# Fourth x casts moved to the middle of a unit, shares moved a unit later, row-sum epsilon moved to ScalarE: an attention + expert + SoLU kernel

## The chip, the cores and the metric

The kernel runs on one core of a Trainium2 chip. The metric is the device time of one execution in microseconds (us), lower is better. TensorE does the matrix products, VectorE and ScalarE read its results from PSUM, GpSimd works on SBUF alone, and SyncE issues all of the transfers.

## The reference

Three stages, in fp32, one behind the other. Batch 4, 8 heads, 576 positions, head size 64; so 2304 tokens of width 512.

```python
# attention, block-causal with blocks of 64
scores = scale * q @ k.T ; scores = where(block_i >= block_j, scores, -1e9)
attn = exp(scores - max) ; attn = attn / (sum(attn) + 1e-9) ; x = attn @ v
# four experts, F = 1024, weighted by normalised shares
p = domain_probs / (domain_probs.sum(-1) + 1e-9)
for e in range(4): out += p[:, e:e+1] * (relu(x @ w1[e]) @ w2[e])
# SoLU layer
h = x @ w_in ; solu = h * softmax(h) ; ln = layernorm(solu) * g_ln ; out = ln @ w_out
```

## The kernel before

**Numbers in two parts.** Every operand of a matrix product is held as a high part (a cast, made by ScalarE in most places) and a low part (value less high part, made by GpSimd or VectorE). A product is then three matmuls: high x high, low x high, high x low.

**Attention.** 16 steps, one for each pair of heads. In step p TensorE turns (transposes) the exponentials of pair p, multiplies them by the values, and makes the scores of pair p + 1. VectorE takes the row maxima, the low parts of the turned tiles, and scales the outputs of pair p - 1 by the inverse row sums (`scale_right`, `scale_left`). ScalarE takes the exponentials (each of the nine row blocks leaves its row sums in one column of `sums`, read back by a small instruction of its own behind the exponential) and the high parts. The inverse sums go this way: `floor_sums` adds 1e-9 to `sums` (L1217), `invert_sums` takes the reciprocal into `rinv_wide` (L1221), TensorE turns `rinv_wide` behind the second turned tile (T8R, L1598), ScalarE copies it out (`copy_rt`, L915), SyncE stores it and loads it back spread over all partitions as `r_sb`, which the scaling waits for. On VectorE the order at the start of step p is `floor_sums(p)`, `scale_right(p - 1, .., 0)`, `invert_sums(p)`, then the maxima of block 8. On ScalarE a step ends with the exponentials of blocks 2, 3 and 0 and `late(p)`, which holds a cast of w1 or x in some steps; the next begins with the high part of the first turned tile (T8) and `copy_rt`.

**Experts.** 4 experts x 3 groups of 768 tokens (sg) x 4 quarters of F (u) = 48 units, m = 0 to 47. The up product of a unit is a Strassen-like scheme of seven products `m1, m6, m2, m7, m5, m4, m3` (6 matmuls each); each takes one sum of w1 and one sum of x (B21, B22, B11, T3, T1, T2, T4), and their results are combined by VectorE and ScalarE into c11, u2, u3, c22, c21, c12. In program order TensorE does m1, m6, m2 of unit m, the four down products of unit m - 1 (36 matmuls), then m7, m5, m4, m3 of unit m. `m6` of the next unit waits until c12 is combined, `m2` for ScalarE's copy of m1 (`m1_copied`; the tiles are `m_a` and `m_b`), `m4` until u3 is there. On VectorE c12 comes behind the low part of c22, and that behind ScalarE's high part of c22.

**The sums of x.** They are made once for each sg and both halves t, in four rounds r of one or two sums: (B21, B22), (B11, T3), (T1, T2), (T4). GpSimd joins x (`x_join`, L761) and adds (`x_add`, L773 to L781); ScalarE casts the high parts of a round (`x_cast`, L935, L948); GpSimd makes the low parts (`x_low_part`, L785). For sg = 0 they are written to `xr` at once. For sg = 1 and 2 they go to one of two buffers `x_tmp` (by r % 2), SyncE stashes them in HBM (`stash_round`, L552) and a cast into a buffer waits until the stash before it has landed (`tmp_stored`). At the start of each sg, SyncE loads the seven sums back into `xr` (`load_operands`, L559), one by one, in the order of the products, each when its stash has landed and the product of the unit before has read the old one. SyncE works through one list in order: (1,0) rounds 0 and 1, w2 loads, the stashes of sg 0's own sums (`stash_first`, seven of 768 KB, in two lots), (1,0) rounds 2 and 3, the rows of x for (2,0), (1,1) rounds 0 to 3, the loads for unit 4, the rows for (2,1), the eight stashes of sg 2, the loads for unit 8.

**Where the casts stand before.** In ScalarE's program for a unit, e = 0, sg < 2: u = 1 behind the copy of c11: (sg+1, 0) rounds 0 and 1. u = 2 behind the copy of m1: (sg+1, 0) rounds 2 and 3; u = 2 at the end: (sg+1, 1) rounds 0 and 1. u = 3 behind the copy of m1: (sg+1, 1) rounds 2 and 3. `after_c11` (L1064) makes the w2 casts of the unit first.

**The shares.** `normalise_probs` (L1353): seven small VectorE operations on 128x18 to 128x72 values, each waiting for the one before, in unit 1 between the w2 low parts and u3. `accumulate` reads the shares from unit 4 on.

Of the kernel before, what the change touches and what calls it, by code (L numbers as in the profile page):

```python
# [16 lines left out]
def build_program(nc, q, k, v, domain_probs, w1, w2, w_in, w_out, g_ln, out):  # L17
# [3 lines left out]
    ALU = mybir.AluOpType  # L21
    ACT = mybir.ActivationFunctionType
# [23 lines left out]
    EPS = 1e-9  # L46
    LN_EPS = 1e-6
    SCALE = 1.0 / DH ** 0.5
    BLOCKS = SEQ // BLOCK
# [92 lines left out]
    with ctx:  # L142
# [78 lines left out]
        sums = put("sums", [P, BLOCKS])  # L221
        sums_e = put("sums_e", [P, BLOCKS])
# [101 lines left out]
        exped = sem("exped")  # L324
# [3 lines left out]
        sums_ready = sem("sums_ready")  # L328
        rinv_made = sem("rinv_made")
# [566 lines left out]
        def _(act):  # L896
            def exp_scores(b, n):
                act.wait_ge(maxed, BLOCKS * n + through_group(group_no(b)))
                if not (isinstance(n, int) and n == 0):
                    act.wait_ge(turned, NT * (n - 1) + last_turn(b) + 1)  # L900
                    if b == 8:
                        act.wait_ge(sums_ready, n)
                target = pr[b][:, 0:keys(b)]
                if b == 8:
                    target = target.rearrange("p (b x) -> p b x", b=2)
                act.activation(target, score_view(b), ACT.Exp, bias=neg_max[:, score_no(b):score_no(b) + 1],  # L906
                               accum_out=sums[:, b:b + 1]).then_inc(exped, 1)

            def high(i, p, par):
                act.wait_ge(turned, NT * p + i + 1)  # L910
                act.activation(turn_target(i, 0), turn_source(i, par), ACT.Copy).then_inc(high_done, 1)
# [65 lines left out]
            def late(p):  # L977
                if p in (0, 2, 4, 6):
                    w1_cast_plain(0, p // 2, 1)
                if p == 11:  # L980
                    x_cast(0, 0, 3)
                if p in (13, 14):
                    x_cast(0, 1, 3 * (p - 13))

            def step(p, par, ahead=True):
                n = p + 1
                high(T8, p, par)
                copy_rt(p, par)
                high(T8R, p, par)
                exp_scores(8, n)  # L990
                high(T67, p, par)
                middle(p)
                high(T67B, p, par)
                exp_scores(7, n)
                high(T45, p, par)
                exp_scores(6, n)
                high(T452, p, par)
                nearly_late(p)
                exp_scores(5, n)
                if ahead:  # L1000
                    key_high(p + 2, par)
                exp_scores(1, n)
                exp_scores(4, n)
                high(T0123, p, par)
                exp_scores(2, n)
                exp_scores(3, n)
                exp_scores(0, n)
                late(p)

            def last_step(p, par):  # L1010
# [27 lines left out]
            key_high(1, 1)  # L1038
            for b in SCORE_ORDER:
                exp_scores(b, 0)  # L1040
            for p in range(PAIRS - 1):
                step(p, p % 2, ahead=p < PAIRS - 2)
            last_step(PAIRS - 1, 1)
# [20 lines left out]
            def after_c11(e, sg, u):  # L1064
                nx = next_w2(e, sg, u)
                if nx:
                    split2(nx[0], 2 * nx[1], gained=nx[0] == EXPERTS)
                    split2(nx[0], 2 * nx[1] + 1, gained=nx[0] == EXPERTS)
                if e == 0 and sg < 2 and u == 1:
                    x_cast(sg + 1, 0, 0)  # L1070
                    x_cast(sg + 1, 0, 1)
                nx = next_w1(e, sg, u)
                if nx:
                    w1_cast_sums(*nx)

            def unit(e, sg, u):
                m = HALF_F * (SUPERS * e + sg) + u
                if m >= 1:
                    copy_m1(m)
                    after_m1(e, sg, u)  # L1080
                hid_c11(m)
                if m >= 1:
                    after_c11(e, sg, u)
                hid_rest(m, "c22", 2, u3[:, :])
                hid_rest(m, "c21", 1, m1(m))
                hid_rest(m, "c12", 3, u2[:, :])
                if e == 0 and sg < 2 and u == 2:
                    x_cast(sg + 1, 1, 0)
                    x_cast(sg + 1, 1, 1)

            for e in range(EXPERTS):
                for sg in range(SUPERS):
# [105 lines left out]
        def _(dve):  # L1198
# [15 lines left out]
                                         in1=k_h[slot][:, :].bitcast(f32), op0=ALU.mult, op1=ALU.subtract  # L1214
                                         ).then_inc(k_split, 1)

            def floor_sums(p):  # L1217
                dve.wait_ge(exped, BLOCKS * (p + 1))
                dve.tensor_scalar(sums_e[:, :], sums[:, :], EPS, None, ALU.add).then_inc(sums_ready, 1)

            def invert_sums(p):  # L1221
                dve.wait_ge(sums_ready, p + 1)
                dve.reciprocal(rinv_wide[:, 0:BLOCKS], sums_e[:, :]).then_inc(rinv_made, 1)  # L1223
# [16 lines left out]

            def step(p, par, first=False, ahead=True):
                n = p + 1
                floor_sums(p)
                if not first:
                    scale_right(p - 1, 1 - par, 0)
                invert_sums(p)
                max_scores(8, n)
                low(T8, p, par)
                if not first:
                    scale_right(p - 1, 1 - par, 1)  # L1250
                low(T8R, p, par)
                max_scores(7, n)
                if not first:
                    scale_left(p - 1, 1 - par)
                low(T67, p, par)
                max_scores(6, n)
                low(T67B, p, par)
                max_scores(5, n)
                low(T45, p, par)
                max_scores(1, n)  # L1260
                max_scores(4, n)
                low(T452, p, par)
                max_scores(2, n)
                max_scores(3, n)
                if ahead:
                    key_low(p + 2, par)
                max_scores(0, n)
                low(T0123, p, par)
# [53 lines left out]
                dve.tensor_tensor(u3[:, :], bank_y(m), m1(m), ALU.add).then_inc(comb_done, 1)  # L1322

            def last_step(p, par):
                floor_sums(p)
                scale_right(p - 1, 1 - par, 0)
                invert_sums(p)
                low(T8, p, par)
                scale_right(p - 1, 1 - par, 1)
                low(T8R, p, par)  # L1330
                scale_left(p - 1, 1 - par)
                low(T67, p, par)
                low(T67B, p, par)
                low(T45, p, par)
                make_u2(0)
                low(T452, p, par)
                low(T0123, p, par)
                scale_right(p, par, 0)
                scale_right(p, par, 1)
                split2(0, 0)  # L1340
                split2(0, 1)
# [40 lines left out]
            def unit(e, sg, u):  # L1382
                n = SUPERS * e + sg
                m = HALF_F * n + u
                if m >= 1:
                    make_u2(m)
                if n >= 1 and u == 1:
                    accumulate(n - 1, 1, downs(m - 2, 4))
                hid_low(m, "c11", 0, bank_x(m))
                nx = next_w2(e, sg, u)  # L1390
                if nx and m >= 1:
                    split2(nx[0], 2 * nx[1], gained=nx[0] == EXPERTS)
                    split2(nx[0], 2 * nx[1] + 1, gained=nx[0] == EXPERTS)
                if n >= 1 and u == 0:
                    if n == 1:
                        for i in range(2):
                            dve.wait_ge(x_stored[i], 16 * PAIRS)
                    if n == 2:
                        dve.wait_ge(x_low, NR * 2 * SUPERS)
                        for s in range(2):  # L1400
                            dve.wait_ge(tmp_stored[s], 16 * 4 * (SUPERS - 1))
                    accumulate(n - 1, 0, downs(m - 1, 2))
                if m == 1:
                    normalise_probs()
                make_u3(m)
                if m == 0:
                    scale_left(PAIRS - 1, 1)
                dve.wait_ge(prod_done, made(m, "m5"))
                dve.wait_ge(comb_done, combined(m, "u3"))
                dve.tensor_tensor(u3[:, :], bank_x(m), u3[:, :], ALU.add).then_inc(comb_done, 1)  # L1410
                dve.wait_ge(prod_done, made(m, "m4"))
                dve.tensor_tensor(m1(m), bank_y(m), m1(m), ALU.add).then_inc(comb_done, 1)
                hid_low(m, "c22", 2, u3[:, :])
                dve.wait_ge(prod_done, made(m, "m3"))
                dve.tensor_tensor(u2[:, :], bank_x(m), u2[:, :], ALU.add).then_inc(comb_done, 1)
                hid_low(m, "c21", 1, m1(m))
                hid_low(m, "c12", 3, u2[:, :])
# [535 lines left out]
```

## Time and profile before

| | us |
|---|---|
| median of 3 runs | 1171.48 (1171.28 to 1173.45) |
| profiled execution, its own time | 1173.69 |
| its span | 1171.9 |
| TensorE busy | 1143.4 (98%) |
| VectorE busy | 645.2 (55%) |
| ScalarE busy | 425.4 (36%) |
| GpSimd busy | 414.7 (35%) |
| granted clock, mean | 0.997 |

Busy time is an average over stages: in the attention stage (up to about 190 us) all four engines are busy most of the time, behind it TensorE alone is. In the rows, PE is TensorE, PEld its weight loads, DVE VectorE, ACT ScalarE, POOL GpSimd, SP SyncE with its DMA queue. Times are us from the start of the span.

### The profile page before, as it was taken

To read this page: it belongs to the slowest core of one execution; us is meant where nothing else is said; L and a number is where in the kernel's file an instruction comes from. 1 tells how busy PE (TensorE), PEld (TensorE's weight loads), DVE (VectorE), ACT (ScalarE), POOL (GpSimd) and SP (SyncE) were. 2 spreads that over 40 slices of the span, in tenths; PEclk is the share of its full clock that TensorE was granted. 3 is DMA by queue.
4 is the path that set the end of the run, shared out by engine and by line. 5 is a ranking of instruction groups with operands and counts; after the bars stand their busy time and mean duration, and the time that the engine had idled before them with its cause. 6 is when DMAs were issued, how large, how long until landed. Compare 5 with 4: busy or idle time off the path is not lost.

```text
span 1171.9 us, 16745 instructions
## 1 busy us (share of the span) xinstructions
PE 1143.4 (98%) x6131; PEld 1021.0 (87%) x6131; DVE 645.2 (55%) x1155; ACT 425.4 (36%) x927; POOL 414.7 (35%) x403
## 2 busy tenths in 40 slices
PE   8999998989989999999999999999999999999998
PEld 7999888879879999999999999999999987888887
DVE  8999997634234533334443434343434368766775
ACT  7888885222213211113321112321112344434432
POOL 7998896652424300004400003410002454442330
PEclk9999999999999999999999999999999999999999
DMA  4766666983472304071504043422225100000000
GB/s 140 218 206 198 211 228 199 368 309 143 143 270 101 142 17 172 1 260 55 207 1 188 1 160 119 151 92 81 109 81 198 37 18 10 28 19 27 19 27 36
DMA packets 68341, 146.28 MB, mean 125 GB/s; under 512 B 6064, under 2 KB 34736, under 8 KB 68272
## 3 DMA queue, kind: packets, MB, share of 16 engines
q1 hardware_dynamic: 68272, 145.36, 35.7%
q8 instruction: 43, 0.70, 0.3%
q14 instruction: 26, 0.21, 0.1%
HBM read 114.60 MB, written 30.74 MB: 124 GB/s over the span
## 4 chain that ended last, share of the span: by engine, by line
PE 75%; DVE 1%; POOL 1%; DMA 1%; issue 0%; ACT 0%; ACTq 0%; POOLq 0%
PE s L1724 34%; PE outp L1585 19%; PE s L1585 10%; PE ring L1585 10%; PE ring L1855 1%; PE s L1798 1%; DMA xr<-x_stash 1%; POOL x_late L761 0%; DMA x_stash<-x_tmp 0%; POOL yop_l L863 0%; DVE yop_l L1433 0%; ACT y_t L1103 0%; DVE acc L1379 0%; POOL x_tmp L785 0%; DVE ex L1505 0%
## 5 line engine op out<-in xcount | busy, mean ns | idle before, releaser
L1724 PE MATMUL s<-xr,w1s 128*128 128x384 f32 x2016 | 363.4, 338 | 11.2 <-issue 6.3
L1724 PEld LDWEIGHTS s<-xr,w1s 128*128 128x128 f32 x2016 | 352.8, 189 | 17.8 <-issue 7.9
L1053 ACT ACTIVATE hid_h<-u 128x384 fp32r<-128x384 f32 x96 | 50.5, 526 | 375.6 <-DVE u L1410 350.6
L720 POOL TENSOR_TENSOR work<-work 128x256 f32<-128x256 f32 x20 | 15.9, 796 | 395.2 <-DMA work<-in_moe_w 269.3
L1365 DVE SCALAR_TENSOR_TENSOR hid_l<-s,hid_h 128x384 fp32r<-128x384 f32 x48 | 26.8, 557 | 134.4 <-ACT hid_h L1049 134.4
L1724 PE MATMUL s<-w1s,yop_h 128*128 128x512 f32 x252 | 85.7, 399 | 1.8 <-POOL yop_l L863 0.7
L1049 ACT ACTIVATE hid_h<-s 128x384 fp32r<-128x384 f32 x48 | 23.5, 490 | 154.9 <-PE s L1585 154.9
L1585 PE MATMUL s<-k_h,qb 128*128 128x288 f32 (+8 forms) x320 | 75.8, 324 | 3.9 <-ACT pr L906 1.9
L1322 DVE TENSOR_TENSOR u<-s,m_b 128x384 f32<-128x384 f32 x24 | 13.4, 558 | 118.7 <-PE s L1724 118.7
L906 ACT ACTIVATE pr<-s,neg_max 128x576 f32<-128x576 f32 (+2 forms) x144 | 75.5, 534 | 4.6 <-DVE neg_max L1201 4.4
L1585 PE MATMUL outp<-w_h,hid_h 128*128 128x512 f32 x192 | 75.4, 393 | 0.0
L1585 PE MATMUL s<-w_h,hid_h 128*128 128x512 f32 x192 | 75.2, 392 | 0.0
L1585 PE MATMUL s<-w_l,hid_h 128*128 128x512 f32 x192 | 75.0, 391 | 0.0
L1585 PE MATMUL outp<-w_l,hid_h 128*128 128x512 f32 x192 | 74.9, 390 | 0.0
L1585 PE MATMUL s<-w_h,hid_l 128*128 128x512 f32 x192 | 74.7, 389 | 0.0
L1585 PE MATMUL ring<-w_h,hid_h 128*128 128x512 f32 x192 | 74.7, 389 | 0.0
L1585 PE MATMUL ring<-w_h,hid_l 128*128 128x512 f32 x192 | 74.7, 389 | 0.0
L1585 PE MATMUL ring<-w_l,hid_h 128*128 128x512 f32 x192 | 74.7, 389 | 0.0
L1585 PE MATMUL outp<-w_h,hid_l 128*128 128x512 f32 x192 | 74.6, 389 | 0.0
L1596 PE MATMUL ring<-ident,pr 128*128 128x128 f32 x400 | 64.9, 280 | 5.8 <-DVE rinv_wide L1223 4.8
L1322 DVE TENSOR_TENSOR u<-s,m_a 128x384 f32<-128x384 f32 x24 | 13.4, 558 | 97.1 <-PE s L1724 97.1
L1201 DVE TENSOR_REDUCE neg_max<-s 128x1 f32<-128x576 f32 (+2 forms) x144 | 65.3, 473 | 0.9 <-PE s L1585 0.8
(172 smaller groups left out, 2455.8 us busy)
## 6 DMA issues: line engine op xcount, KB each, us to landing
xr<-x_stash SPq DMA_DIRECT2D x77, 768.0 KB, 6.3
r_sb<-r_scratch SPq DMA_DIRECT2D x16, 576.0 KB, 4.2
x_rows<-x_n SPq DMA_DIRECT2D x32, 288.0 KB, 4.6
work<-x_rows SPq DMA_DIRECT2D x24, 384.0 KB, 6.6
x_stash<-x_tmp SPq DMA_DIRECT2D x12, 768.0 KB, 3.9
work<-in_moe_w SPq DMA_DIRECT2D x32, 256.0 KB, 4.2
stage<-in_moe_w SPq DMA_DIRECT2D x32, 256.0 KB, 5.0
x_stash<-xr SPq DMA_DIRECT2D x7, 768.0 KB, 9.6
```

The source lines that it names most:

```text
L720: pool.tensor_tensor(s1, a21, a22, ALU.add).then_inc(w1_sums, 1)
L906: act.activation(target, score_view(b), ACT.Exp, bias=neg_max[:, score_no(b):score_no(b) + 1], accum_out=sums[:, b:b + 1]).then_inc(exped, 1)
L1049: act.activation(hid[0][0][:, :], bank_x(m), ACT.Relu).then_inc(hid_high, 1)
L1053: act.activation(hid[slot][0][:, :], source, ACT.Relu).then_inc(hid_high, 1)
L1201: dve.tensor_reduce(neg_max[:, score_no(b):score_no(b) + 1], score_view(b), AX.XY if b == 8 else AX.X, ALU.max, negate=True).then_inc(maxe ...
L1322: dve.tensor_tensor(u3[:, :], bank_y(m), m1(m), ALU.add).then_inc(comb_done, 1)
L1365: dve.scalar_tensor_tensor(out=hid[slot][1][:, :], in0=source, scalar=0.0, in1=hid[slot][0][:, :].bitcast(f32), op0=ALU.max, op1=ALU.subtr ...
L1585: last = pe.matmul(target, x, y, start=start and i == 0, stop=stop and i == 2)
L1596: last = pe.transpose(slot[:, at * P:(at + 1) * P], pr[b][:, j * P:(j + 1) * P], ident[:, :])
L1724: last = pe.matmul(target, x, y, start=start and i == 0, stop=stop and i == 2, skip_group_check=True)
L1798: last = pe.transpose(s01[:, 512 * i + d * P:512 * i + (d + 1) * P], acc[:, t * D + d * P:t * D + (d + 1) * P], ident[:, :])
L1855: last = pe.transpose(ring[:, f * P:(f + 1) * P], ex[i % 2][:, f * P:(f + 1) * P], ident[:, :])
```

## The change

Three moves; every operation is still done as often as before.

```diff
@@ ScalarE, attention
+            def floor_sums(p):
+                act.wait_ge(exped, BLOCKS * (p + 1))
+                if not (isinstance(p, int) and p == 0):
+                    act.wait_ge(rinv_made, p)
+                act.activation(sums_e[:, :], sums[:, :], ACT.Copy, bias=EPS).then_inc(sums_ready, 1)
@@ def step: behind exp_scores(0, n), ahead of late(p); and once behind the first pair's exponentials
+                floor_sums(n)
@@ ScalarE, after_c11
-                if e == 0 and sg < 2 and u == 1:
-                    x_cast(sg + 1, 0, 0)
-                    x_cast(sg + 1, 0, 1)
+                if e == 0 and sg < 2 and u in (1, 2):
+                    x_cast(sg + 1, u - 1, 0)
+                    x_cast(sg + 1, u - 1, 1)
@@ ScalarE, end of unit
-                if e == 0 and sg < 2 and u == 2:
-                    x_cast(sg + 1, 1, 0)
-                    x_cast(sg + 1, 1, 1)
@@ VectorE, attention
-            def floor_sums(p):
-                dve.wait_ge(exped, BLOCKS * (p + 1))
-                dve.tensor_scalar(sums_e[:, :], sums[:, :], EPS, None, ALU.add).then_inc(sums_ready, 1)
@@ VectorE, first line of step and of last_step
-                floor_sums(p)
@@ VectorE, unit
-                if m == 1:
+                if m == 2:
                     normalise_probs()
```

## Rows read from the trace of the kernel before

**Rows 1.** Stretches: each engine's busy us (instructions), granted clock, DMA share, GB/s.
```profile
326.00:328.00 2.00, 2.00 (x7) 1.63 (x7) 0.00 (x0) 0.49 (x1) 0.00 (x0) 0.50 1.03 430
420.00:1105.00 685.00, 682.56 (x3410) 605.51 (x3409) 323.83 (x559) 186.07 (x327) 150.05 (x155) 1.00 0.24 87
```
**Rows 2.** Who waited for whom, whole span: us in total, times, longest.
```profile
PE s L1724 <- issue: 6.3, 2, 3.7
PE ring L1596 <- DVE rinv_wide L1223: 4.8, 8, 1.1
PE s L1724 <- ACT m_b L1027: 1.9, 2, 1.0
```
**Rows 3.** Chain that ended last, 195 to 420 us: start, us, what.
```profile
242.45 3.78 POOL x_late L761 x3
...
251.65 6.15 DMA xr<-x_stash
...
269.71 7.28 PE s L1724 x42
...
321.55 3.74 issue
325.29 5.05 PE s L1724 x18
...
369.50 7.28 PE s L1724 x42
...
384.98 7.30 PE s L1724 x42
```
**Rows 4.** Timeline, units 2 to 4: start, us, engine, line, what [idle before, releaser].
```profile
232.41 6.40 PE L1724 MATMUL s<-xr,w1s 128*128 128x384 f32 x36
...
235.28 0.53 ACT L1053 ACTIVATE hid_h<-u 128x384 fp32r<-128x384 f32 x1 [7.20 <-DVE u L1410]
...
237.79 1.56 ACT L948 ACTIVATE x_tmp<-x_late 128x768 fp32r<-128x768 f32 x2
...
238.70 3.62 POOL L785 TENSOR_TENSOR x_tmp<-x_late,x_tmp 128x768 fp32r<-128x768 f32 x2 [7.04 <-ACT x_tmp L948]
...
239.78 1.31 PE L1724 MATMUL s<-xr,w1s 128*128 128x384 f32 x6 [0.97 <-ACT m_b L1027]
...
257.85 3.69 PE L1724 MATMUL s<-xr,w1s 128*128 128x384 f32 x12 [0.55 <-DMA xr<-x_stash]
```
**Rows 5.** Timeline of ScalarE, unit 6.
```profile
303.38 0.53 ACT L1053 ACTIVATE hid_h<-u 128x384 fp32r<-128x384 f32 x1 [8.24 <-DVE u L1410]
...
305.89 1.56 ACT L948 ACTIVATE x_tmp<-x_late 128x768 fp32r<-128x768 f32 x2
```
**Rows 6.** The two stashes (1, 0) of rounds 2 and 3, by tile.
```profile
L555 SPq DMA_DIRECT2D x_stash<-x_tmp x2: 370/566/761, 225.6 to 226.6; - x2
...
DMA to landing us min/median/max: 11.1/11.1/11.1
```
**Rows 7.** Timeline, unit 1: the shares and what follows.
```profile
214.12 4.12 DVE L1360 TENSOR_TENSOR probs_n<-probs_raw,probs_sum 128x18 f32<-128x18 f32 x4
...
218.89 5.48 PE L1724 MATMUL s<-xr,w1s 128*128 128x384 f32 x30 [1.21 <-DVE u L1322]
```
**Rows 8.** Timeline of the attention stage, at the epsilon and the inverses.
```profile
26.15 0.27 ACT L915 ACTIVATE rt_sb<-ring 9x128 f32<-9x128 f32 x1 [0.53 <-PE ring L1598]
...
128.54 0.49 DVE L1238 TENSOR_TENSOR x_n<-outp,r_sb 128x320 f32<-128x320 f32 x1 [0.54 <-DMA r_sb<-r_scratch]
...
173.87 1.85 POOL L785 TENSOR_TENSOR xr<-t_first,xr 128x768 fp32r<-128x768 f32 x1
...
173.93 1.82 DVE L1219 TENSOR_SCALAR sums_e<-sums 128x9 f32<-128x9 f32 x1 [0.46 <-ACT pr L906]
...
176.41 0.30 PE L1596 MATMUL ring<-ident,pr 128*128 128x128 f32 x1 [0.79 <-DVE rinv_wide L1223]
...
189.77 1.29 PE L1724 MATMUL s<-xr,w1s 128*128 128x384 f32 x6 [0.91 <-POOL xr L785]
```

More of the change, by code:

```diff
@@ L1040, in _ @@
                 exp_scores(b, 0)
+            floor_sums(0)
             for p in range(PAIRS - 1):
@@ L1324, in last_step @@
             def last_step(p, par):
-                floor_sums(p)
                 scale_right(p - 1, 1 - par, 0)
```

## The prediction, made before the changed kernel was seen

> **What bounds the kernel now.** I read the stretches first. From 420 to 1105 us TensorE is busy 682.56 of 685 us at the full clock [rows 1]: nothing that this change touches can shorten the work there, and one unit of the expert stage is 15.48 us (384.98 less 369.50) [rows 3]. So the change can only win or lose where TensorE waits. The list of TensorE's waits gives those places [rows 2]: 6.3 us in two idle times with no visible releaser, 4.8 us for the inverted sums (`rinv_wide`) in the attention stage, 1.9 us in two waits for a ScalarE copy `m_b`. The chain of waits places the first: the operand loads at the starts of units 4 and 8, each of which hangs on a line cast of x -> GpSimd's low parts -> stash -> reload [rows 3]. The granted clock is the last view: at 326 to 328 us it is 0.50, the 1.2 GHz level [rows 1], after an idle time of 3.74 us.
>
> What the two restarts cost, before: at unit 4, 0.97 us for `m_b` [rows 4], 0.55 us before the second product, 2.57 us before the first (6.3 less 3.74 [rows 2, 3]; unit 3 had ended at 253.45), and 12 matmuls in 3.69 us. At the full clock 12 take 2.08; the lower clock costs 1.6. At unit 8: the other 0.9 of the `m_b` waits [rows 2], 3.74 idle, and 18 matmuls in 5.05 where 3.12 is due: 1.9. That is 5.7 and 6.6 us [rows 2 to 4]. (A stretch of the chain with 42 matmuls is 7.28 us, so one is 0.173.)
>
> **The change part by part.**
>
> (a) *The fourth pair of x casts (sg+1, t=1, rounds 0 and 1) goes from the end of unit 2 to its middle*, behind the two w2 casts and ahead of the three hidden copies. Work is the same: two casts in 1.56 us [rows 4]. What matters is when its semaphores come, and what is queued behind it on ScalarE, which works in order.
>
> At the second restart (unit 6, making x for unit 8) the middle is free: ScalarE waits 8.24 us for the hidden copy at 303.38, and the casts come at 305.89 [rows 5]. The cast needs the stashes of rounds 2 and 3 landed; these are issued near 293.5 and 294.6 and a stash takes 3.6 to 5.6 us there, so about 297 to 300. The casts are then done by 299 to 301, before ScalarE is wanted. GpSimd's 3.6 us of low parts, the stashes, the round-2 cast in unit 7 (which waited for a stash until 314.3) and the loads all move up by some 6 us; the first operand is in by about 317 and the second by 319 to 321, where TensorE comes for them at 320.3 and 321.3. I take all three items as gone: -6.6. The bounds are -6.9 (with the slow restart after each idle time) and -4 (the second operand about a microsecond late, and the clock falls anyway).
>
> At the first restart (unit 2, making x for unit 4) the middle is not free. The cast of round 0 needs the stash of (1, 0, 2) and that of round 1 the stash of (1, 0, 3). They are issued at 225.6 and 226.6 and land 11.1 us later each, at 236.7 and 237.7 [rows 6], as they stand behind seven 768 KB stashes. Before, the casts started at 237.79, past both; now ScalarE stops at the first of them from about 227 on. The copy of c22, which it made at 235.28 [rows 4], is behind it in the queue. With the 1.2 us of (b) TensorE is earlier: unit 3 starts at 232.41 + 24 x 0.173 = 236.57 before, 235.3 now, and its first product ends at 236.4. Its second (`m6`) needs c12, which VectorE adds only after c22's low part. The chain: cast 236.7 to 237.5, cast 237.7 to 238.5, copy of c22 to 239.05, low part to 239.6, c12 to 240.1 (each of the three some 0.55 us). So TensorE, which lost 0.97 us here, now idles about 3.7 us. That is as long as the 3.74 us that pulled the clock to 0.50 [rows 1, 3], so I count a fall here: +1.9. Unit 3's remaining work, from 241.0 to 253.45 before (12.4 us), starts at 242.2: it ends at 254.6, or 256.5 with the lower clock.
>
> And the loads? GpSimd gets the round-0 cast at 237.6 instead of 238.70 [rows 4], 1.1 us earlier; the chain from there (join of x at 242.45, last load 251.65 to 257.80 [rows 3]) moves by as much, the second operand lands at 256.7. TensorE, held up, arrives at 256.5, wants it at 257.6 and does not wait; no fall of the clock there. Unit 5 starts at 256.5 + 15.48 = 272.0, before it was 269.71 + 4.16 = 273.87 [rows 3]: -1.9 with (b) in it. If the clock does not fall in unit 3, the landing at 256.7 decides: 256.7 + 14.4 = 271.1, -2.8. If it falls twice: 0.
>
> (b) *The shares (`normalise_probs`) go from unit 1 to unit 2.* In unit 1 four of its seven small operations take 4.12 us and TensorE waits 1.21 us for the u3 behind them [rows 7]. In unit 2 VectorE starts them near 228.5; GpSimd's 1 us sums of x end at 231.7 and then GpSimd has nothing until the casts. I expect the shares done near 232.5, u3 started as its product comes, no wait. Gain in unit 1: 1.2, already spent in (a), where what comes next is late; bounds 0 and 1.3 for that term.
>
> (c) *The epsilon of the row sums goes from VectorE to ScalarE*, 16 times. Before: the last exponential's sum is read, VectorE adds (0.17 us where nothing is beside it, up to 1.82), scales (0.48), inverts (0.20), and TensorE waits 0.79 us at 176.41 [rows 8]. Now VectorE scales before the sums are there; ScalarE adds in some 0.3 us: the nearest row is its copy of 9x128, 0.27 us [rows 8], plus its wait for its own last write. The inversion comes 0.25 to 1.9 us earlier. Of TensorE's eight waits [rows 2] (0.40, 0.49, 0.47, 1.09, 0.34, 0.33, 0.79, 0.91 in order; one stands in [rows 8]), those at 129.3 and 164.3 stay, since the scaling, at 128.54, waited for the loaded inverses (`r_sb`) [rows 8]. The last two (0.79, 0.91) give nothing: from 166 us on GpSimd works without a pause to the last low part of x, for which the first expert product waits at 189.77 [rows 8]; TensorE would only wait longer there. That leaves 0.40 + 0.49 + 0.47 + 0.34 = 1.7: -1.7. On ScalarE the add costs about 0.3 us and the sum's read-back; behind it are the late cast and the copy of the first turned tile, and then ScalarE idles anyway for the inverses' transpose, 0.53 us at the least [rows 8]. Bounds: -4.8 (all of [rows 2]'s item) and +4.8 (16 x 0.3, if nothing covers it). I take -1.7, near the rows that say who waits.
>
> The 1.82 us add at 173.93 ran while GpSimd had a 1.85 us operation from 173.87, and ended just behind it [rows 8]. The Trainium skill (SBUF — State Buffer, section SBUF: two separate sides) says that VectorE in a two-port mode and GpSimd lock one pair of ports for whole instructions, while ScalarE never waits for anyone. By that rule the add's long forms vanish on ScalarE and don't pass on to the inversion; my sum has it so, and without it the inversion would inherit some of the delay, about -1. Against the move, the Trainium skill (ScalarE: Activation LUTs, Rules for kernel authors) says to put `add` on VectorE, not ScalarE; what that would do is rival D.
>
> **Sum**, against the profiled execution (span 1171.9, its own time 1173.7): -6.6 - 1.9 - 1.7 = -10.2: span 1161.7, time 1163.5. The median of the runs, 1171.48, is 2.2 below that execution; the same difference from it gives **1161.3 us**.
>
> **Rivals.**
>
> A. *The block in unit 2 is mild, or the attention stage gains all.* No fall of the clock there (-0.9) and up to -3 more from (c): 1157.5 to 1160.4. For: the first fall came behind two idle times with one product between; attention's slow steps are slow on VectorE too. Against: 3.7 us is as long as the idle time before the second fall.
>
> B. *The block costs more than it gives*: a second fall at unit 4, or landings a microsecond later: the first restart gives 0 or loses 1, with the rest as forecast: 1163.2 to 1164.3. For: the DMA engines are full there, the landing is fixed by them and not by ScalarE.
>
> C. *The second restart keeps half of its wait*: the second operand comes late and the clock falls: -4 in place of -6.6, or -2: 1163.9 to 1165.9. Against: nothing else is in the DMA queue there.
>
> D. *Slower: ScalarE becomes the attention stage's bound.* Place: between the last exponential and the copy of the turned inverses. Price: wait for its own sum (0.4, what VectorE waited for it), the add 0.27 and a lost overlap of 0.1, 0.75 us a step, in 15 steps 11.3 us; with -8.5 from the rest and nothing of the -1.7: 1174.3. It decides where ScalarE's idle time before the inverses is under 0.75 us; the smallest is 0.53 [rows 8], but most steps have over 1.
>
> E. *Nothing of (a) arrives*: if the operand loads' start is set by the order on SyncE's queue and not by the casts, only (c) stays: 1169.8. Against: the chain [rows 3] runs through the GpSimd join and the stash.
>
> **How the numbers follow.** Forecast 0.50, A 0.22, B 0.12, C 0.09, D 0.04, E 0.03. Range 1157 to 1165.5: it takes in A, B, and most of C. 0.2% is 2.3 us, about what a measurement of this kernel can tell: all but D, and a mix of E with losses (0.01), are faster. Faster 0.94, same 0.02, slower 0.04.
>
> **What would show it.** Right: no idle time of TensorE at units 7 and 8, no 0.50 clock there; the casts of unit 6 near 299 less the shift; in unit 2 ScalarE waiting for `x_stash<-x_tmp` to about 236 and TensorE idle 3 to 4 us before `m6` of unit 3, with a fall of the clock behind it; no wait for u3 in unit 1 or 2; TensorE's wait for `rinv_wide` at 2 to 3.5 us, and a longer one for x before the first expert product. Wrong: idle time on TensorE before the first product of unit 4 or 8 of over 1 us; ScalarE never idle before the inverses' transpose; steps of the attention stage longer than the 11.1 us of the quick ones now.

## The result, and the profile after

The changed kernel took 1159.86 us in the median of 4 runs (1159.10 to 1160.79), the kernel before 1172.30 us in 4 runs beside it (1171.28 to 1173.45): a ratio of 0.9894, 95% interval 0.9877 to 0.9911. A second set of 4 runs gave 0.9887 (0.9867 to 0.9908). The forecast was 1161.3 us, range 1157 to 1165.5.

The profiled execution took 1159.74 us, its span is 1157.9; TensorE is busy 1138.7 us, VectorE 633.4, ScalarE 428.5, GpSimd 415.7, mean granted clock 0.999. The span is 14.0 us shorter, the median 12.4: the execution that the prediction was made against was among the longer ones of its kernel.

The chain of waits from 195 us on (start, us, what), which answers to [rows 3]:

```profile
235.37 4.24 POOL x_late L761 x3
...
241.44 3.55 DMA x_stash<-x_tmp
...
245.44 7.41 DMA xr<-x_stash
...
262.41 7.28 PE s L1723 x42
277.89 7.28 PE s L1723 x42
...
308.85 7.30 PE s L1723 x42
324.34 7.28 PE s L1723 x42
```

One row of 42 matmuls stands for one unit. They now follow each other every 15.48 us right through units 7 and 8, where before 3.74 us of issue and a slow stretch lay between. Three marks divide the gain: A, the start of the first expert product (the last row of [rows 8], 189.77 before); R5, the first row of 42 matmuls in this chain (269.71 before; unit 5 starts 4.16 behind it); R9, the same one turn later (338.54 before, 324.34 now).

| | before | after | change | forecast |
|---|---|---|---|---|
| A (attention) | 189.77 | 185.31 | -4.46 | -1.7 |
| A to R5 (first restart, shares) | 79.94 | 77.10 | -2.84 | -1.9 |
| R5 to R9 (second restart) | 68.83 | 61.93 | -6.90 | -6.6 |
| sum | | | -14.20 | -10.2 |

The list of TensorE's waits, whole span (us in total, times, longest), answers to [rows 2]: the issue and `m_b` lines are gone, a new one leads.

```profile
PE s L1723 <- DVE u L1414: 2.5, 1, 2.5
PE ring L1595 <- DVE rinv_wide L1224: 1.7, 3, 0.9
...
PE ring L1595 <- DVE ptr_l L1213: 1.6, 2, 0.9
...
PE s L1723 <- POOL xr L785: 1.5, 1, 1.5
```

The timeline of units 2 to 4 (start, us, engine, line, what, idle before and releaser) shows where the new wait comes from; it answers to [rows 4, 7].

```profile
223.43 0.22 DVE L1355 TENSOR_REDUCE probs_sum<-probs_raw 128x18 f32<-128x72 f32 x1
...
224.75 1.41 DVE L1359 TENSOR_TENSOR probs_n<-probs_raw,probs_sum 128x18 f32<-128x18 f32 x4
...
226.19 5.37 PE L1723 MATMUL s<-xr,w1s 128*128 128x384 f32 x30
227.50 0.56 DVE L1322 TENSOR_TENSOR u<-s,m_a 128x384 f32<-128x384 f32 x1 [1.33 <-PE s L1723]
...
230.41 1.79 ACT L954 ACTIVATE x_tmp<-x_late 128x768 fp32r<-128x768 f32 x2 [8.55 <-DMA x_stash<-x_tmp]
...
232.10 0.51 ACT L1061 ACTIVATE hid_h<-u 128x384 fp32r<-128x384 f32 x1
...
232.64 0.92 DVE L1364 SCALAR_TENSOR_TENSOR hid_l<-u,hid_h 128x384 fp32r<-128x384 f32 x1 [2.58 <-ACT hid_h L1061]
233.48 0.55 DVE L1414 TENSOR_TENSOR u<-s,u 128x384 f32<-128x384 f32 x1
...
234.08 3.76 PE L1723 MATMUL s<-xr,w1s 128*128 128x384 f32 x12 [2.53 <-DVE u L1414]
```

The last four of the shares' seven operations take 1.41 us in place of 4.12, and no TensorE wait for u3 follows. ScalarE stands 8.55 us at the moved casts, with the copy of c22 (232.10) behind them; VectorE has to wait for that copy (2.58), c12 comes at 233.48, and TensorE idles 2.53 us before `m6`. That is the block forecast in step (a), and the clock falls behind it, as the stretches show (columns as in [rows 1]):

```profile
234.00:236.00 2.00, 1.92 (x6) 1.92 (x7) 2.00 (x3) 0.90 (x2) 1.87 (x2) 0.50 0.99 356
236.00:238.00 2.00, 2.00 (x10) 1.95 (x9) 1.76 (x2) 0.85 (x1) 2.00 (x2) 0.71 1.02 369
326.00:328.00 2.00, 2.00 (x14) 2.00 (x13) 1.06 (x3) 0.52 (x1) 0.00 (x0) 1.00 0.12 43
```

The attention stage, as the stretch 5 to 185 us (before, then after):

```profile
5.00:185.00 180.00, 170.84 (x1276) 159.41 (x1274) 168.82 (x340) 149.36 (x438) 154.73 (x141) 1.00 0.63 197
```

```profile
5.00:185.00 180.00, 171.76 (x1298) 162.72 (x1297) 162.65 (x332) 155.56 (x465) 159.73 (x144) 1.00 0.65 202
```

VectorE is busy 6.2 us less, ScalarE 6.2 more, and TensorE has issued 22 more matmuls by the same moment. The add by tile (ns min/median/max), before and after, with the inversion after:

```profile
L1219 DVE TENSOR_SCALAR sums_e<-sums x16: 174/608/1820, 13.4 to 186.4; 128x9 f32<-128x9 f32 x16
```

```profile
L913 ACT ACTIVATE sums_e<-sums x16: 211/212/213, 13.4 to 181.9; 128x9 f32<-128x9 f32 x16
L1224 DVE RECIPROCAL rinv_wide<-sums_e x16: 204/215/219, 13.6 to 182.2; 128x9 f32<-128x9 f32 x16
```

On VectorE the add took anything from 0.17 to 1.82 us; on ScalarE it takes 0.21 each time, and the inversion did not inherit the long forms. The Trainium skill (SBUF — State Buffer, section SBUF: two separate sides) says that VectorE in a two-port mode and GpSimd keep each other out for whole instructions, and that ScalarE waits for neither; both rows agree. VectorE still waits for ScalarE's add, 3.6 us in 14 times, in place of the 6.0 us in 16 times that it waited for the last exponential.

### The profile page after: what moved, and what is told of

It is laid out like the page before. It is cut to its first block, busy times and chain, and to the rows that moved or that the text cites. A ratio compares the mean times of both kernels' runs of the same rounds, so it can differ in the third digit from the quotient of the medians.

```text
span 1157.9 us, 16760 instructions
## 1 busy us (share of the span) xinstructions
PE 1138.7 (98%) x6131; PEld 1020.9 (88%) x6131; DVE 633.4 (55%) x1139; ACT 428.5 (37%) x943; POOL 415.7 (36%) x403
## 4 chain that ended last, share of the span: by engine, by line
PE 76%; POOL 1%; DVE 1%; DMA 1%; ACT 0%; issue 0%; SPq 0%; ACTq 0%; POOLq 0%
PE s L1723 34%; PE outp L1584 19%; PE s L1584 11%; PE ring L1584 10%; PE ring L1854 1%; DMA xr<-x_stash 1%; PE s L1797 1%; POOL x_late L761 0%; DMA x_stash<-x_tmp 0%; POOL yop_l L863 0%; DVE yop_l L1432 0%; ACT y_t L1108 0%; DVE acc L1378 0%; POOL x_tmp L785 0%; DVE ex L1504 0%
## 5 line engine op out<-in xcount | busy, mean ns | idle before, releaser
L906 ACT ACTIVATE pr<-s,neg_max 128x576 f32<-128x576 f32 (+2 forms) x144 | 75.5, 537 | 3.3 <-DVE neg_max L1206 3.0
L1584 PE MATMUL outp<-w_h,hid_h 128*128 128x512 f32 x192 | 75.5, 393 | 0.0
```

Of the source, the lines that this page charges most:

```text
L1584: last = pe.matmul(target, x, y, start=start and i == 0, stop=stop and i == 2)
```

## The experiments

Each ran beside the kernel before. Ratios are against it, with 95% intervals; A, A to R5 and R5 to R9 come from one trace of each kernel.

| kernel | median us | ratio | A | A to R5 | R5 to R9 |
|---|---|---|---|---|---|
| before | 1172.3 | | 189.77 | 79.94 | 68.83 |
| after | 1159.9 | 0.9894 (0.9877 to 0.9911) | 185.31 | 77.10 | 61.93 |
| e1_eps | 1168.9 | 0.9972 (0.9959 to 0.9985) | 186.19 | 79.69 | 69.69 |
| e2_cast | 1163.7 | 0.9925 (0.9904 to 0.9946) | 187.90 | 79.31 | 61.93 |
| e3_shares | 1171.0 | 0.9991 (0.9976 to 1.0005) | 188.62 | 77.72 | 68.72 |
| e4_order | 1169.6 | 0.9975 (0.9964 to 0.9987) | 186.32 | 79.79 | 69.63 |
| e5_second_only | 1160.6 | 0.9897 (0.9881 to 0.9914) | 184.29 | 79.80 | 61.93 |
| e6_stash_ahead | 1160.7 | 0.9899 (0.9878 to 0.9921) | 184.05 | 79.70 | 61.95 |
| e7_hold_all | 1162.6 | 0.9915 (0.9898 to 0.9931) | 183.53 | 81.76 | 61.94 |
| e8_double | 1158.4 | 0.9879 (0.9862 to 0.9895) | 185.75 | 77.19 | 61.91 |
| e9_rows_ahead | 1158.9 | 0.9875 (0.9854 to 0.9896) | 185.78 | 76.64 | 61.93 |
| e10_rows_first | 1160.9 | 0.9889 (0.9870 to 0.9907) | 185.65 | 78.91 | 61.94 |
| e11_after_again | 1159.7 | 0.9887 (0.9867 to 0.9908) | 184.35 | 77.06 | 61.93 |
| e12_late_two | 1156.8 | 0.9865 (0.9838 to 0.9892) | 184.69 | 73.25 | 61.91 |

### One part alone: e1_eps, e2_cast, e3_shares

Each is the kernel before with one of the three moves of the diff and nothing else. The marker lines of the edits:

```diff
+                floor_sums(n)                                    # e1: add on ScalarE, and off VectorE
+                if e == 0 and sg < 2 and u in (1, 2):            # e2: casts in the middle of u = 2
+                if m == 2:                                       # e3: shares in unit 2
```

> Only the move of the epsilon add to ScalarE. Theory: VectorE's in-order queue paces the attention steps, and the add held it twice (wait for the last exponential, then up to 1.8 us beside GpSimd), so every later operation of the step moves up, not only the inversion. The first expert product then starts near 185.3 us, 4.5 earlier than the 189.77 of the kernel before, and the two restarts of the expert stage cost what they did: unit 9 starts about 4.5 earlier than 342.70, the time is 4 to 5 us below the kernel before. Rival (the prediction's own term): only the waits for the inverted sums go, 1.7 us, the rest of the shift was chance: first product at 188.1, time 1.7 below.

> Only the fourth casts in the middle of a unit. Theory: the second restart is gone (unit 8 to unit 9 is 15.48 us, no idle time, 6.9 us gained). In unit 2 ScalarE waits for the stashes, to about 236.7; TensorE is 1.2 us later there than with the shares moved, so it idles about 2.5 us before m6 of unit 3. Its first restart is set by the landing of the loads as in the full change: unit 5 starts 1 to 3 us before 273.87. In all 8 to 10 us below the kernel before. Rival: the shares' wait in unit 1 comes on top, and the first restart gains nothing: 6.9.

> Only the shares in unit 2. Theory: unit 1 loses its 1.21 us wait, but the stashes' landing and the casts behind it set the restart at unit 4, so TensorE gives back most of it there: unit 5 starts 0 to 1 us before 273.87 and the time is within 1 us of the kernel before. Rival: the 1.2 us is kept to the end, 1.2 to 1.3 us below.

The second restart belongs to the casts alone: R5 to R9 is 61.93 us (four units of 15.48) with them, 68.7 to 69.7 without. The first restart adds up: -0.63 with the casts alone, -2.22 with the shares alone, -2.84 with both. Each of these is one trace, and the clock's falls differ between them, so that they add up to 0.01 us is luck. The casts alone gave 0.75%, 8.8 us, in the 8 to 10 that I had expected; the time of the shares alone can't be told from no change. With the casts alone TensorE's wait for u3 in unit 1 stays:

```profile
PE s L1721 <- DVE u L1412: 2.2, 2, 2.1
PE s L1721 <- DVE u L1319: 1.2, 1, 1.2
```

The epsilon alone is worth 0.28%, 3.3 us, with an interval of 1.8 to 4.8 us: less than the 4 to 5 that I had expected, more than the rival's 1.7. e1's waits for the inverses fall as after's do:

```profile
PE ring L1598 <- DVE rinv_wide L1227: 2.1, 3, 0.9
```

A varies from trace to trace: 185.31 and 184.35 for the changed kernel itself, and 183.5 to 186.2 over all that have its attention stage. The three traces with the add on VectorE ahead of the scaling have 189.77, 187.90 and 188.62, mean 188.8; the ten with it on ScalarE have a mean of 185.0. So move (c) is worth 3.8 us in the traces and 3.3 in the times, and some 0.7 of the 4.46 in the table is chance.

### Engine or order: e4_order, e8_double

```diff
 # e4: kernel before, both step functions of VectorE; the add stays on VectorE
-                floor_sums(p)
                 scale_right(p - 1, ..., 0)
+                floor_sums(p)
                 invert_sums(p)
 # e8: changed kernel, ScalarE; sums_d is a new tile that nobody reads
+                act.activation(sums_d[:, :], sums[:, :], ACT.Copy, bias=EPS)
                 act.activation(sums_e[:, :], sums[:, :], ACT.Copy, bias=EPS).then_inc(sums_ready, 1)
```

> The kernel before with the add left on VectorE but put behind the first scaling (scale_right h = 0) instead of ahead of it. Theory: the early scaling uses the time in which VectorE waited for the last exponential (0.33 to 0.46 us a step, 6.0 us in all), but the add still waits for GpSimd's operations: about half of the epsilon move's gain, first expert product at 187 to 188.5. Rival A (order is all): as the move to ScalarE, 185.3. Rival B (the engine is all): 189.8, as before.

> The changed kernel with ScalarE's epsilon add made twice (the first into a tile that nobody reads). Theory: ScalarE waits for the turned inverses in each step, so one more operation of 0.21 us there delays only the inversion by 0.1 to 0.2 us a step; first expert product within 1 us of 185.3 to 186.2, time 0 to 1.5 us above the changed kernel. Rival D of the prediction (ScalarE paces the steps): 16 x 0.2 = 3.3 us above.

The order alone, with the add on VectorE, gives 0.25% (0.13% to 0.36%) and A = 186.32: most of what (c) gives, where I had expected half and A at 187 to 188.5. What cost time was VectorE standing in front of the add until the last exponential's sums were there, with the scaling, which needs none of them, queued behind. VectorE's waits say so, of before and then of e4:

```profile
DVE sums_e L1219 <- ACT pr L906: 6.0, 16, 0.5
```

```profile
DVE sums_e L1219 <- ACT pr L906: 0.6, 1, 0.6
PE ring L1596 <- DVE rinv_wide L1223: 3.9, 5, 2.0
```

TensorE's listed wait for the inverses fell by only 0.9 us (4.8 to 3.9), and the adds on VectorE still took up to 1.12 us (median 0.547). What the engine adds to the order is too small to be told here (0.28% against 0.25%, with wide intervals). A second add in each of 16 steps costs nothing that shows (A 185.75, inside the spread of the others, and a time 1.5 us under the changed kernel's). Rival D, a price of 0.75 us a step, is refuted: ScalarE has that room. The Trainium skill (ScalarE: Activation LUTs, section Rules for kernel authors) says to put an add on VectorE; the quickest add there, 0.174 us against 0.212 on ScalarE, agrees in direction, but beside GpSimd the VectorE form had a median of 0.608, and the kernel with the add on ScalarE is the faster one.

e8 also shows the clock. Its TensorE idled 2.67 us before the same `m6`, longer than after's 2.53, and the granted clock stayed at 1.00 (stretch 234 to 236):

```profile
234.69 2.36 PE L1725 MATMUL s<-xr,w1s 128*128 128x384 f32 x12 [2.67 <-DVE u L1416]
```

```profile
234.00:236.00 2.00, 1.30 (x7) 1.31 (x8) 2.00 (x3) 0.90 (x2) 1.87 (x2) 1.00 0.73 273
```

The same 12 matmuls take 2.36 us here and 3.76 in after, and A to R5 is 77.19 against 77.10; in e11, the changed kernel run again, TensorE idles 1.48 us before `m6`, the clock does not fall, and A to R5 is 77.06. The fall in unit 3 is worth nothing, since what it delays TensorE by, TensorE then doesn't wait for the loads. In e8 these waits stand at unit 4:

```profile
249.64 1.28 PE L1725 MATMUL s<-xr,w1s 128*128 128x384 f32 x6 [0.23 <-issue]
251.55 1.30 PE L1725 MATMUL s<-xr,w1s 128*128 128x384 f32 x6 [0.63 <-DMA xr<-x_stash]
253.43 1.32 PE L1725 MATMUL s<-xr,w1s 128*128 128x384 f32 x6 [0.57 <-DMA xr<-x_stash]
```

where after has one of 0.58 us.

### Is the block worth having: e5_second_only, e6_stash_ahead, e7_hold_all

```diff
 # e5: changed kernel, ScalarE: the moved casts only for sg = 1; for sg = 0 they stay at the end of unit 2
-                if e == 0 and sg < 2 and u in (1, 2):
+                if e == 0 and sg < 2 and (u == 1 or (sg, u) == (1, 2)):
 # e6: changed kernel, SyncE's list
-            stash_first(range(3, NP))
+            stash_first(range(3, 5))
             stash_round(1, 0, 2)
             stash_round(1, 0, 3)
+            stash_first(range(5, NP))
 # e7: as e6, but all four (3 to NP) go behind
```

> The changed kernel with the fourth casts of the first restart (sg = 0) back at the end of unit 2; those of the second stay in the middle. Theory: in the middle of unit 2 the casts win about as much on the loads as the blocked ScalarE costs: without the block TensorE's 2.5 us idle time before m6 of unit 3 becomes 0.97 us before m2, and the fall of the clock comes behind the idle time at unit 4, as in the kernel before. Unit 5 starts 77.5 to 78 us after the first expert product (77.10 + 4.16 in the changed kernel), the time is 0 to 1 us above the changed kernel. Rival: the block was pure loss, 2 to 3 us below the changed kernel. The second restart stays free, 61.93 us between the marks at units 5 and 9.

> The changed kernel with the two stashes of (1, 0) rounds 2 and 3 put ahead of the last two 768 KB stashes of sg 0's own sums in SyncE's list. Theory: ScalarE's block in unit 2 is the time that these stashes stand in the DMA queue; two stashes less in front are about 3.7 us, so ScalarE waits about 5 us, ends before the copy of c22 is wanted, TensorE has no idle time before m6 of unit 3 and no fall of the clock, and the loads for unit 4 come 2 to 3.5 us earlier. 3 to 5 us below the changed kernel. Rival: SyncE now waits for the low parts before it issues the last two, the DMA engines run empty for that time, and the same bytes land later: the loads for unit 4 are as late as before, gain 0 to 1 us.

> As the run before, but all four of the last stashes of sg 0's sums stand behind the two of (1, 0). Theory: the block is gone altogether, but the DMA engines have nothing for about 5 us around unit 1's end and the four stashes (3 MB, 7.5 us) run into the rows for (2, 0) and the stashes of (1, 1), so the loads for unit 4 are later than in the run before: 1 to 4 us below the changed kernel, less than the run before. Rival: only the landing of the two counts: as good as the run before or better.

e5 has no block, and its first restart is as slow as before's: 0.97 us idle for `m_b`, 2.61 before unit 4, 0.54 before the second product, and the next 12 matmuls at the lower clock. A to R5 is 79.80 us, where I had expected 77.5 to 78. So the block, which idles TensorE 2.5 us, is no loss. How much it buys is less sure than 79.80 against 77.10 makes it look: from unit 4's first product to R5 this trace takes 15.20 us and before's 13.69, with a like wait inside (0.54 and 0.55), because the lower clock lasted some 3.4 us longer, to past 256 us (the stretches are in the last section). By that estimate 1.5 of the 2.7 us is the clock's. In the medians it is 0.7 us, inside the spread.

e6 takes most of the block away and gains nothing. The timeline of its ScalarE and GpSimd:

```profile
225.33 1.83 ACT L955 ACTIVATE x_tmp<-x_late 128x768 fp32r<-128x768 f32 x2 [4.71 <-DMA x_stash<-x_tmp]
226.26 3.67 POOL L786 TENSOR_TENSOR x_tmp<-x_late,x_tmp 128x768 fp32r<-128x768 f32 x2 [1.19 <-ACT x_tmp L955]
235.18 3.79 POOL L762 TENSOR_TENSOR x_late<-work 128x512 f32<-128x512 f32 x3 [5.25 <-DMA work<-x_rows]
```

The cast comes 5.1 us earlier than in after (3.8 counted from A), and TensorE idles 0.5 us before `m6`. But GpSimd's join of x for (2, 0), the start of the chain to the loads, now waits 5.25 us for its rows, which stand in the same queue behind the two postponed stashes. It starts at A + 51.1, in after at A + 50.1. (A to R5, 79.70, holds the same long fall of the clock as e5's: 15.16 us from unit 4's first product to R5, behind 2.96 us of idle time.) In e7, where all four postponed stashes stand ahead of the rows, that wait is 9.32 us, and the median is 2.7 us above the changed kernel's; 1.9 of the 4.7 us by which its A to R5 is longer is a fall of the clock at A, before the edit acts (last section). I had expected 3 to 5 us under the changed kernel for e6 and 1 to 4 for e7. For e6 its rival came: loads as late as in after, and no gain. The gain that a shorter block was to bring came in neither; the next wait was in the same full queue (DMA share 0.99 and 1.02 in the stretches of after above).

### The queue's order: e9, e10, e11, e12

e9, e10 and e12 are the changed kernel with another order in SyncE's list; e11 is the changed kernel itself on the chip of e9 and e10. The new order is shown, two or three calls on a line:

```diff
 # e9
+            stash_first(range(3, 5)); stash_round(1, 0, 2); stash_round(1, 0, 3)
+            load_x(2, 0)
+            stash_first(range(5, NP))
 # e10
+            load_x(2, 0)
+            stash_first(range(3, 5)); stash_round(1, 0, 2); stash_round(1, 0, 3)
+            stash_first(range(5, NP))
 # e12
+            stash_first(range(3, 5)); stash_round(1, 0, 2); stash_round(1, 0, 3)
+            load_x(2, 0)
+            stash_round(1, 1, 0); stash_round(1, 1, 1)
+            stash_first(range(5, NP))
+            stash_round(1, 1, 2); stash_round(1, 1, 3)
```

> The changed kernel itself, timed again on the chip of the two kernels beside it. Both theories: ratio near 0.989 (1158.5 to 1161 us); the marks R5 - A near 77 us (up to 80 with a longer fall of the clock at unit 3 or 4), R9 - R5 61.9 us.

> SyncE's list: the stashes (1,0) of rounds 2 and 3 and the rows of x for (2,0) stand ahead of the last two of sg 0's own stashes. Theory (the first restart is set by what lands last in a full DMA queue: first the two stashes for ScalarE's casts, then the rows of (2,0) for GpSimd's join): both come earlier now and what comes later is two stashes that nobody needs before 243 us. ScalarE's wait in unit 2 falls from 8.6 to about 5 us, GpSimd's join starts without the 5 us wait that it had with the stashes alone ahead, near A + 47 to 48 instead of A + 50.1, TensorE idles under 1 us before m6 of unit 3 and under 1 us before unit 4, and R5 - A is 75 to 76 us: 1 to 2 us under the changed kernel (1158 to 1159 us). Rival (the whole chain goes at the pace of the queue whatever its order): the two late stashes, or the later transfers that share the queue with them, are late in turn, the first reload waits for them, and R5 - A stays at 77 to 80 us, the time within 1 us of the changed kernel.

> As e9, but the rows for (2,0) stand ahead of the second lot of sg 0's stashes altogether, so ahead of the stashes (1,0) of rounds 2 and 3 as well. Theory: they are in by about A + 40, the join has them long before it is free; the stashes of rounds 2 and 3 land about as in e9 or up to 1 us later; R5 - A 75 to 76.5 us. Rival (pace of the queue): R5 - A 77 to 80 us.

> As e9 (the stashes (1,0) of rounds 2 and 3 and the rows for (2,0) ahead of the last two of sg 0's own stashes), and those two go once more behind the stashes (1,1) of rounds 0 and 1. Theory (in e9 the next wait is ScalarE's, 4.7 us for the landing of the stash (1,1,0), which took 8.25 us behind those two): now it lands in some 4 us, the cast of (1,1) round 2 starts near A + 48 to 49 instead of A + 52.2, the first reload near A + 55 instead of A + 58.5, R5 - A is 74 to 75.5 us and the time 1 to 2 us under e9's 1158.9. Rival (the queue's total is what counts: the first reload must wait for all seven of sg 0's stashes anyway): the two late ones land near A + 56 to 58, the first reload starts no earlier than in e9, R5 - A 76.5 to 77.5 us, the time as e9.

e9 does what was wanted with the first two waits and meets a third: the join starts at A + 46.5, but the cast of (1, 1) round 2 waits for a stash that now takes 8.25 us behind the two postponed ones. Its chain:

```profile
229.65 8.25 DMA x_stash<-x_tmp
...
237.98 0.86 ACT x_tmp L955
```

A to R5 is 76.64, 0.4 us under after, between the theory's 75 to 76 and the rival's 77 to 80. TensorE idles 2.11 us before unit 4, where the theory had under 1; the time, 1158.9, fits both. In e10 the rows first make the block nearly as long as in after (8.01 us). Its A to R5 is 1.8 us longer than after's, but TensorE was 1.85 us behind already at A + 27.25 (A + 25.40 in after), before the edited part of the list acts, for its clock fell at A (last section). Without that, e10 would be as after by my estimate, and my 75 to 76.5 missed. e12 puts the two stashes where nobody waits behind them. Chain and waits of TensorE from 195 us on:

```profile
224.35 6.07 DMA work<-x_rows
230.49 4.54 POOL x_late L764 x3
...
236.86 3.56 DMA x_stash<-x_tmp
...
240.86 7.52 DMA xr<-x_stash
...
257.94 7.28 PE s L1726 x42
```

```profile
PE s L1726 <- DMA xr<-x_stash: 0.3, 1, 0.3
PE s L1726 <- DVE u L1417: 0.2, 1, 0.2
```

ScalarE's wait in unit 2 is 4.41 us, TensorE's before `m6` 0.23, and before unit 4's third product 0.34: A to R5 is 73.25 us, 3.9 under after and better than the 74 to 75.5 expected, without a fall of the clock. So the rival, that only the queue's total counts, is out. At 1156.8 us it has the lowest median here (1155.2 to 1158.8, against 1158.7 to 1160.8 in the changed kernel's eight runs, which did not run beside it). The ratios' intervals overlap (0.9838 to 0.9892, against 0.9867 to 0.9908), so the time alone does not settle the gain; the trace shows where it is. The bytes are the same, only their order in a queue that is full differs.

## Why the prediction was right, point by point

The time came 1.4 us under the forecast, well inside its range, and the sign of every step held. The sizes did not all hold, and that the time came so near is in part luck: the gain was 12.4 us where 10.2 was forecast, and the kernel before had a median 0.8 us higher in these runs than in those that the forecast started from.

- **(a), second restart, -6.6: right.** -6.90 in the trace, with (a) alone as with all. The casts of unit 6 start at 289.97 (305.89 before), no idle time and no 0.50 clock at unit 8; rivals C and E are out.
- **(a), block in unit 2: mechanism right, size off.** Forecast: ScalarE held until the stashes land, TensorE idle 3.7 us before `m6`, clock down behind it. Measured 2.53, and the clock down in this trace, up in e8 and e11. The landings were taken as fixed at 236.7 and 237.7; but SyncE's list is itself paced by the units, so they moved with A (4.5 us) and 1.8 more: the first of the two was issued at A + 34.1 (A + 35.8 before), and the casts started at A + 45.10, where A + 46.9 had been reckoned. And I charged the fall with 1.9 us; it is worth nothing here (77.10 with it, 77.19 and 77.06 without), as the landing of the loads decides. The -2.84 equals my own -2.8 for "the landing decides", but by luck: I had the second operand of unit 4 decide, and it was the third (TensorE's 0.58 us wait at 252.90); and most of the -2.84 is the shares'.
- **(b), "gain already spent in (a)": wrong.** With the shares alone the first restart is 2.22 us shorter, with the casts alone 0.63: the shares bring most of that -2.84. The step that failed is the fixed landing: the transfers before the chain to the loads are issued as the units go, 1.7 us earlier from A in e3 as in after, and so what is won in unit 1 is not lost at a landing. TensorE's marks divide e3's 2.22 us: 0.22 is there when `m7` of unit 1 starts (A + 25.66 before, A + 25.44 in e3), from a gap near A + 15 us, ahead of the shares; 1.72 when `m7` of unit 2 starts (A + 42.64 and A + 40.92), with the 1.21 us wait in between, 1.77 at unit 4's first product (A + 66.25 and A + 64.48), and the last 0.45 comes there, as this row of e3 has no wait of 0.55 us before the second product:

```profile
253.10 5.04 PE L1724 MATMUL s<-xr,w1s 128*128 128x384 f32 x18 [2.51 <-issue]
```

No wait for u3 came in unit 1 or 2, as forecast.
- **(c), epsilon, -1.7: the mis-sized term.** It measured -3.3 to -3.8. The step that failed is the sum over TensorE's waits for `rinv_wide`: 0.40 + 0.49 + 0.47 + 0.34. That list counts where TensorE's wait is put down to the inverses; VectorE, busy 168.8 of 180 us, paced the steps, and its 6.0 us in front of the add held up everything behind it, also where TensorE's waits are put down to others. e4 shows it: with the add still on VectorE and only that wait gone, TensorE's listed wait falls by 0.9 us and the time by 0.25%, 2.9 us. That VectorE also has 6.2 us less to do in the changed kernel may count for the rest; no run tells the two apart within the noise. Of the signs named for it, ScalarE's add came at 0.21 us (0.3 forecast), the waits for `rinv_wide` at 1.7 us, a little under the 2 to 3.5 named, and the wait for x rose from 0.91 to 1.49, as expected. And "the last two give nothing" held: GpSimd's last 23 us before A are the same in both traces, and the gain was all made by the time they begin:

```profile
166.48 0.72 POOL L708 CAST v_hl<-v_nat 128x640 fp32r<-128x640 f32 x1 [0.96 <-DMA v_nat<-in_v]
```

```profile
161.95 0.72 POOL L708 CAST v_hl<-v_nat 128x640 fp32r<-128x640 f32 x1 [1.32 <-DMA v_nat<-in_v]
```

(Before, then after: 4.53 us apart, where A is 4.46 apart.)

Rival A (block mild or attention gains all, 1157.5 to 1160.4) describes the outcome better than the forecast does: the time lies in its span, attention gained more, and the restart came at its better end. Rival B is refuted by the marks and by e5, rival D by e8.

## What to carry to other kernels

A list of waits says where the pacing engine is late, not how much it paces. For an edit on an engine that is busy over 90% of a stage, take the listed waits as the lower end (1.7 us here) and that engine's saved time as the upper (6.2 us of busy time here); the gain, 3.3 to 3.8, lay between. An instruction that has to wait, ahead of work that is ready, costs its wait as well as its time: swapping the two gave most of the gain. A landing read from the trace is not a fixed time when its issue depends on the work that the edit moves. And when a wait hangs on a transfer in a full queue, list everything that is wanted from that queue with the time when it is wanted: moving one or two transfers passed the wait on (e6, e7, e9), putting all in the order of need left 0.6 us of TensorE's idle time there (e12).

## What the runs showed of the hardware

After idle times of nearly one length TensorE's clock did three things: idle 2.53 us, down to 0.50 (after); idle 2.67, stays at 1.00 (e8); idle 2.61, down, and still at 0.50, the 1.2 GHz level, five microseconds on (e5, stretches of unit 4; e6 does the same behind 2.96):

```profile
250.00:252.00 2.00, 1.46 (x6) 1.27 (x5) 0.00 (x0) 0.49 (x1) 0.00 (x0) 0.51 1.01 424
252.00:254.00 2.00, 2.00 (x8) 1.90 (x7) 0.56 (x1) 0.00 (x0) 0.00 (x0) 0.50 1.01 424
254.00:256.00 2.00, 2.00 (x6) 1.73 (x6) 0.00 (x0) 0.00 (x0) 0.00 (x0) 0.50 1.03 430
```

It did two things at one and the same place, too, the first expert product, behind the same 1.49 us: in after, e5, e9, e11 and e12 six matmuls take 1.28 or 1.29 us, in e10 and e7 they take 2.26, with a granted clock of 0.50 behind (186 to 188 us in e10, 184 to 186 in e7). After, then e10:

```profile
185.31 1.28 PE L1723 MATMUL s<-xr,w1s 128*128 128x384 f32 x6 [1.49 <-POOL xr L785]
```

```profile
185.65 2.26 PE L1724 MATMUL s<-xr,w1s 128*128 128x384 f32 x6 [1.49 <-POOL xr L786]
```

The long fall makes 1.5 us more than the short one in a single trace, the fall at A 1.85; what decides between them was not found. So a difference of 1 to 2 us between two traces says nothing until their clocks are compared.
